# Batches 1 to 3: k is transposed inside the score passes, by a unit matrix beside the high part of q, and the channel mixer keeps two hidden buffers instead of three

## The reference

```python
def _attn_ref(q, k, v, alpha):
    for t in range(S):
        state = alpha[:, :, t, :, None] * state + np.einsum('bhd,bhe->bhde', k[:, :, t], v[:, :, t])
        y[:, :, t] = np.einsum('bhd,bhde->bhe', q[:, :, t], state)

def _moe_ref(x, w_tok1, w_tok2, w_ch1, w_ch2):      # x: (4, 768, 384)
    h = np.maximum(x.transpose(0, 2, 1) @ w_tok1, 0.0) @ w_tok2      # 768 -> 256 -> 768
    u = x + h.transpose(0, 2, 1)
    return u + np.maximum(u @ w_ch1, 0.0) @ w_ch2                    # 384 -> 1536 -> 384

def _moe2_ref(x, mu_k, mu_r, w_k, w_v, w_r):
    xk, xr = (mu * x + (1.0 - mu) * x_prev for mu in (mu_k, mu_r))
    k = np.maximum(xk @ w_k, 0.0)
    return 1.0 / (1.0 + np.exp(-(xr @ w_r))) * (k * k @ w_v)
```

## Time and profile before

| | us |
|---|---|
| median of 3 runs | 725.66 |
| lowest and highest | 725.64, 725.91 |
| the profiled execution | 725.77 |
| its span, first to last instruction | 723.8 |
| busy in the span: PE, DVE, ACT, POOL | 718.9, 474.7, 324.6, 199.8 |

### The profile page before, as it was taken

How to read it: one execution, slowest core, us unless ns; L and a number is a source line. 1 busy time by engine, 2 the same in 40 slices (tenths; PEclk the granted TensorE clock), 3 DMA queues, 4 the chain that set the end, 5 groups by cost and what they waited for, 6 DMA issues and landing times.

```text
span 723.8 us, 12708 instructions
## 1 busy us (share of the span) xinstructions
PE 718.9 (99%) x4230; PEld 676.2 (93%) x4230; DVE 474.7 (66%) x1252; ACT 324.6 (45%) x892; POOL 199.8 (28%) x351
## 2 busy tenths in 40 slices
PE   8999999999999999999999999999999999999998
PEld 7999999999999999999999999998888888888898
DVE  8988888865988875888884412348474655647361
ACT  5876554433544442544443231337353543527160
POOL 4876564333343332334432440220000000000000
PEclk9999999999999999999999999999999999999999
DMA  9975535542425544343531323012121112120201
GB/s 205 233 148 83 93 58 111 79 72 67 55 42 86 104 80 69 59 56 58 111 63 24 98 88 121 34 44 77 23 57 24 30 53 35 45 44 1 44 0 44
DMA packets 240751, 50.99 MB, mean 70 GB/s; under 512 B 221936, under 2 KB 237872, under 8 KB 240688
## 3 DMA queue, kind: packets, MB, share of 16 engines
q1 hardware_dynamic: 237408, 45.06, 33.4%
q0 software_dynamic: 1280, 4.72, 1.8%
q10 hardware_dynamic: 2000, 0.41, 0.3%
HBM read 37.17 MB, written 12.98 MB: 69 GB/s over the span
## 4 chain that ended last, share of the span: by engine, by line
PE 98%; DVE 1%; issue 0%; ACT 0%; POOL 0%; DVEq 0%; POOLq 0%
PE bank L879 21%; PE bank L895 21%; PE bank L961 14%; PE bank L983 11%; PE bank L791 5%; PE bank L970 4%; PE bank L759 4%; PE bank L867 4%; PE bank L832 3%; PE bank L1005 2%; PE bank L796 2%; PE bank L789 2%; PE bank L754 1%; PE bank L716 1%; PE bank L848 1%; PE bank L992 1%
## 5 line engine op out<-in xcount | busy, mean ns | idle before, releaser
L1108 ACT ACTIVATE hid_hi<-bank 128x384 fp32r<-128x384 f32 x96 | 47.2, 492 | 117.5 <-PE bank L879 117.4
L1391 DVE SCALAR_TENSOR_TENSOR hid_lo<-bank,hid_hi 128x384 fp32r<-128x384 f32 x96 | 53.3, 555 | 67.9 <-ACT hid_hi L1108 67.1
L879 PE MATMUL bank<-u_hi,wch_hi 128*128 128x384 f32 x288 | 72.0, 357 | 0.0
L879 PE MATMUL bank<-u_lo,wch_hi 128*128 128x384 f32 x288 | 65.9, 336 | 0.0
L895 PE MATMUL bank<-hid_lo,wch_hi 128*128 128x384 f32 x288 | 65.6, 335 | 0.0
L879 PE MATMUL bank<-u_hi,wch_lo 128*128 128x384 f32 x288 | 65.6, 335 | 0.0
L895 PE MATMUL bank<-hid_hi,wch_hi 128*128 128x384 f32 x288 | 65.4, 334 | 0.0
L895 PE MATMUL bank<-hid_hi,wch_lo 128*128 128x384 f32 x288 | 65.4, 334 | 0.0
L625 POOL TENSOR_SCALAR_AFFINE_SELECT relu_k<-relu_k 128x256 f32<-128x256 f32 x72 | 29.5, 409 | 111.2 <-ACT relu_k L1090 111.2
L1081 ACT ACTIVATE x_hi<-bank 128x96 fp32r<-128x96 f32 x96 | 23.6, 246 | 78.3 <-PE bank L796 65.4
L1305 DVE SCALAR_TENSOR_TENSOR qs_lo<-qkd,rhead,qs_hi 96x128 fp32r<-96x128 f32 x144 | 50.8, 392 | 10.1 <-ACT qs_hi L1102 8.7
(11 more groups left out here) (198 smaller groups left out, 1739.9 us busy)
## 6 DMA issues: line engine op xcount, KB each, us to landing
w_raw<-in_moe_w_ch SPq DMA_DIRECT2D x12, 384.0 KB, 3.7
vt<-in_v SPq DMA_DIRECT2D x48, 72.0 KB, 2.2
x_scratch<-x_sum SPq DMA_DIRECT2D x18, 192.0 KB, 2.1
x_sum<-x_scratch SPq DMA_DIRECT2D x72, 48.0 KB, 2.2
out<-x_half SPq DMA_DIRECT2D x40, 64.0 KB, 1.9
qka_words<-in_alpha SPq DMA_DIRECT2D x49, 48.0 KB, 2.3
qka_words<-in_k SPq DMA_DIRECT2D x49, 48.0 KB, 2.2
qka_words<-in_q SPq DMA_DIRECT2D x49, 48.0 KB, 2.3
```

The costliest lines, as they stand in the source:

```text
L879: mm = nc.tensor.matmul(dst, ch1_w(a, n % KC, jj), u[c][:, n % KC, half * HT:(half + 1) * HT], start=(n == 0), stop=(n == 3 * KC - 1))
L1108: nc.scalar.activation(dst, b_ring[t % 2][:, 0:HT], func).then_inc(tile_hi, 1)
L1391: ins = nc.vector.scalar_tensor_tensor(dst, src, 0.0, hi, ALU.max, ALU.subtract)
```

## The change

`turn_k` is gone. A unit matrix of 96 x 96 is written once by ACT at the start, between the two buffers of q's high part: `qs_hi_unit` holds q of even steps (256 words), the unit matrix (96), q of odd steps (256). In the two passes that have q's high part as the moving operand, the operand is now 352 words wide, q and the unit matrix together: even steps with q first, odd steps with the unit matrix first. The products of k's high and of k's low part with the unit matrix add up in bank 1 to k transposed, beside the scores (columns 0 to 255 and 256 to 351, or, for odd steps, 96 to 351 and 0 to 95). The middle pass, and all three for chunk 5, stay at 256 columns. `scores_done` comes from the last score pass in every step. The hidden buffers are two (HJ = 2); `hid_flat` is declared with 1024 words per part instead of 1152.

```diff
--- before.py
+++ after.py
@@ -42,7 +42,7 @@
     KT = TOK // P
     NJ = CH // P
     NF = FF // P
-    HJ = 3
+    HJ = 2
     TM = HT // P
     UNITS = 2 * NJ
     TILES = KT + 2 * KC + UNITS
@@ -99,7 +99,8 @@
         x = [sb(f"x_{n}", [P, NC, DM], F32R) for n in ("hi", "lo")]
         h1 = [sb(f"h1_{n}", [P, KT, DM], F32R) for n in ("hi", "lo")]
         u = [sb(f"u_{n}", [P, KC, S], F32R) for n in ("hi", "lo")]
-        hid = [sb(f"hid_{n}", [P, HJ, HT], F32R) for n in ("hi", "lo")]
+        hid_flat = [sb(f"hid_{n}", [P, (KC - 1) * UT], F32R) for n in ("hi", "lo")]
+        hid = [words[:, 0:HJ * HT].rearrange("p (j t) -> p j t", j=HJ) for words in hid_flat]
         x2_half = [sb(f"x2_half{n}", [P, KC, HT]) for n in range(2)]
 
 
@@ -113,7 +114,21 @@
         rhead = sb("rhead", [P, 4, 2])
         qkd = sb("qkd", [P, 6, P])
 
-        qs = [sb(f"qs_{n}", [P, 2, 2 * P], F32R) for n in ("hi", "lo")]
+        qs_hi_unit = sb("qs_hi_unit", [P, 2 * 2 * P + W2], F32R)
+        qs_lo = sb("qs_lo", [P, 2, 2 * P], F32R)
+        unit = qs_hi_unit[0:W2, 2 * P:2 * P + W2]
+
+        def qs_of(n, i):
+
+            if n == 1:
+                return qs_lo[0:W2, i % 2, :]
+            first = (2 * P + W2) * (i % 2)
+            return qs_hi_unit[0:W2, first:first + 2 * P]
+
+        def qs_and_unit(i):
+
+            first = 2 * P * (i % 2)
+            return qs_hi_unit[0:W2, first:first + 2 * P + W2]
         ks = [sb(f"ks_{n}", [P, 2, P], F32R) for n in ("hi", "lo")]
         relu_k = sb("relu_k", [P, 2, HT])
         am = relu_k[:, :, 0:2 * P]
@@ -141,7 +156,6 @@
         relu_ring, mixed_ring = ([words[:, :, :].rearrange("p a c -> p (a c)")[:, 0:UT] for words in pair]
                                  for pair in ((relu_k, decays), (mixed, qkd)))
         x_flat = [x[n][:, :, :].rearrange("p a c -> p (a c)") for n in range(2)]
-        hid_flat = [hid[n][:, :, :].rearrange("p a c -> p (a c)") for n in range(2)]
         mix_out = [[[x_flat[n][:, c * UT:(c + 1) * UT] for c in range(KC)] for n in range(2)],
                    [[x_flat[n][:, KC * UT:(KC + 1) * UT]] + [hid_flat[n][:, c * UT:(c + 1) * UT] for c in range(KC - 1)]
                     for n in range(2)]]
@@ -182,7 +196,9 @@
 
         def scores_kdT(r, i):
 
-            b_sc = bank[7] if is_first(r) and i % 2 else bank[1]
+            if not is_first(r) and i % 2:
+                return bank[1][:, W2:W2 + 2 * P], bank[1][:, 0:W2]
+            b_sc = bank[7] if i % 2 else bank[1]
             return b_sc[:, 0:2 * P], b_sc[:, 2 * P:2 * P + W2]
 
         def y_kv(r, i):
@@ -217,6 +233,7 @@
         split_ready = sem("split_ready")
         qkd_ready = sem("qkd_ready")
         scores_done = sem("scores_done")
+        unit_ready = sem("unit_ready")
         am_ready = sem("am_ready")
         am_copied = sem("am_copied")
         ks_lo_ready = sem("ks_lo_ready")
@@ -755,17 +772,15 @@
                 else:
                     pe.wait_ge(split_ready, 2 * (STEPS * (r - 1) + i + 1))
                     pe.wait_ge(ks_lo_ready, STEPS * (r - 1) + i + 1)
+                    if r == 1 and i == 0:
+                        pe.wait_ge(unit_ready, 1)
                     for n, (a, b) in enumerate(PASSES):
-                        mm = nc.tensor.matmul(scores, ks[a][0:W2, i % 2, :], qs[b][0:W2, i % 2, :],
-                                              start=(n == 0), stop=(n == 2))
-                if is_first(r) or c == NC - 1:
-                    mm.then_inc(scores_done, 1)
-
-            def turn_k(r, i):
-
-                if step(r, i)[0] < NC - 1:
-                    nc.tensor.transpose(scores_kdT(r, i)[1], qkd[0:W2, second_of(i), :], ident[0:W2, 0:W2])\
-                        .then_inc(scores_done, 1)
+                        if b == 0 and c < NC - 1:
+                            dst, moving = bank[1][:, 0:2 * P + W2], qs_and_unit(i)
+                        else:
+                            dst, moving = scores, qs_of(b, i)
+                        mm = nc.tensor.matmul(dst, ks[a][0:W2, i % 2, :], moving, start=(n == 0), stop=(n == 2))
+                mm.then_inc(scores_done, 1)
 
             def v_of(r, i):
 
@@ -815,8 +830,6 @@
                     attention_scores(r, sc)
                 if yo is not None:
                     attention_out(r, yo)
-                if sc is not None:
-                    turn_k(r, sc)
 
             def claim(b, t):
 
@@ -1098,7 +1111,7 @@
                     nc.scalar.activation(ks[0][0:W2, i % 2, :], qkd[0:W2, second_of(i), :], ACT.Copy)\
                         .then_inc(ks_hi_ready, 1)
                 for h in range(2):
-                    dst = qbd[:, i % 2, :] if is_first(r) else qs[0][:, i % 2, :]
+                    dst = qbd[:, i % 2, :] if is_first(r) else qs_of(0, i)
                     nc.scalar.activation(dst[0:W2, h * P:(h + 1) * P], qkd[0:W2, first_of(i), :], ACT.Copy,
                                          scale=rhead[0:W2, i % 4, h:h + 1])\
                         .then_inc(qbd_ready, 1)
@@ -1166,6 +1179,8 @@
             for head, stop, loaded in ((2, 4, second_pair_loaded), (4, H, qka_loaded[0])):
                 act.dma_start(qka3[0][1][:, head:stop, 0:D], k[0, head:stop, 0:P, :].rearrange("h p d -> p h d"))\
                    .then_inc(loaded, 16)
+            act.wait_ge(consts_g, 3)
+            nc.scalar.activation(unit, ident[0:W2, 0:W2], ACT.Copy).then_inc(unit_ready, 1)
             for s in range(SLOTS):
                 head_part(s)
                 for j in range(2 * CH1_END):
@@ -1302,8 +1317,8 @@
                 for h in range(2):
                     cols = slice(h * P, (h + 1) * P)
                     dve.wait_ge(qbd_ready, 2 * (STEPS * r + i) + h + 1)
-                    nc.vector.scalar_tensor_tensor(qs[1][0:W2, i % 2, cols], qkd[0:W2, first_of(i), :],
-                                                   rhead[0:W2, i % 4, h:h + 1], qs[0][0:W2, i % 2, cols],
+                    nc.vector.scalar_tensor_tensor(qs_of(1, i)[:, cols], qkd[0:W2, first_of(i), :],
+                                                   rhead[0:W2, i % 4, h:h + 1], qs_of(0, i)[:, cols],
                                                    ALU.mult, ALU.subtract).then_inc(split_ready, 1)
 
             def mask(r, i):
```

## The result

| us | before | changed |
|---|---|---|
| median (9 runs each, same chip) | 725.67 | 727.19 |
| lowest and highest | 725.62, 726.02 | 725.76, 729.09 |
| ratio, 95% interval | | 1.0019, 1.001 to 1.0027 |
| the profiled execution | 725.77 | 725.91 |
| its span | 723.8 | 724.0 |

The changed kernel is 1.52 us slower at the median, just over the 1.45 us (0.2%) that the prediction called no change (by the ratio, 1.0019, just under it). It is above the prediction's range (724.4 to 726.2), and on the other side of zero from its 0.74 us gain. The medians hide a second difference: nine executions of the kernel before lie within 0.40 us, nine of the changed one within 3.33 us. The highest of these, 729.09, also has the lowest granted clock, 0.997; the other eight lie within 1.92 us at 0.999 or more. A sum over PE's instructions can't give such a spread.

The account below looks back on a forecast made before the run. PE's own instructions were taken to bound the kernel. Removing transposes gives 5.66 us, added columns cost 4.92, net 0.74 less: 725.03 from the profiled 725.77, or 724.9 against the median; range 724.4 to 726.2.

Parts of the forecast that it names:

- What else moves: Side effects on waits, buffers, unit matrix and queues: no wait added inside the batches, SP, DVE and POOL queues keep order.
- Rival (D): A stall appears as the output step starts 0.08 later: at worst 4.8 us more, 730; chance 0.02.
- The net of the sum: Transposes removed less columns added in batches 1 to 3: 5.66 - 4.92 = 0.74 us less.
- 42 transposes behind the state product, 0.087 each: Removed transposes that follow L796, the state update: 42 x 0.087 = 3.65 us back.
- 9 behind the heads' output (first chunk), 0.11 each: Removed transposes following L791 in a head pair's first chunk: 0.99 us back, between bounds of 0.087 and 0.115 each.
- 9 in slots without an output step, 1.02 us: Removed transposes directly behind a score pass: 7 x 0.12 + 2 x 0.09 = 1.02 us back.
- The added columns, 0.041 each: 96 more columns on two of three score passes: 120 x 0.041 = 4.92 us more (4.8 to 5.04).
- The third step of batches 2 and 3: The wide first pass fills a 0.07 us hole before the second; some 0.04 either way, twice.
- the clock and the busy share of the batches: In batches 1 to 3 PE is busy throughout, 350 us, at a granted clock of 1.00.
- the two hidden buffers at nothing: ACT's writes to the hidden buffers: PE's order already frees each buffer in time, so two cost nothing.
- the unit matrix at nothing: One ACT copy of 96 x 96 at the start, 0.26 us, covered; 0.3 us once if not.
- the weighing of the rule on weight loads: Skill rules give 42.5 ns (2.4 us more in all) or 107 ns (1.5 less) per transpose; rows lie between.

Follow-up runs that it names:

- experiment 1: The changed kernel again without any edit, for more executions: 727.17 us (725.67 to 727.90, 11 runs), ratio 1.0018.
- experiment 2: The changed kernel with 120 idle instructions on PE (waits long satisfied) in place of the 60 removed transposes: 725.51 us, ratio 0.9997.
- experiment 5: The kernel before with 136 idle instructions on PE, so its blocks begin at the same work as in the changed kernel: 727.29 us, ratio 1.002.
- experiment 3: The kernel before with 120 idle instructions on PE, placed behind the transposes: 725.67 us, ratio 1.0.
- experiment 6: The kernel before with each of the 60 transposes replaced by two idle instructions, leaving out part of the computation: 721.42 us, ratio 0.9941.
- experiment 7: The changed kernel with the transposes kept, so only the wider passes and two hidden buffers are new against the kernel before: 729.91 us, ratio 1.0055.
- experiment 9: The changed kernel with 32 idle instructions on PE, all in batch 1: 725.59 us, ratio 0.9997.
- experiment 4: The kernel before with two hidden buffers instead of three and nothing else: 725.92 us, ratio 1.0002.

## Why the prediction was wrong

**The step that failed** is "What else moves". It went through the queues of the engines and found that SP's, DVE's and POOL's keep their order, and that no wait is added inside the batches. Both are right, but it looked for added waits nowhere else, and put them at nothing. It left out one queue: the one that brings PE's own instructions. Removing 120 of them moves every block transfer of the program, and one came to lie beside a store on whose end DVE, and behind it PE, depend. The kernel before had 0.23 us of cover there (update 16 at 411.637, DVE's tile at 411.87); the page says nothing of so small a margin, and the prediction looked for the thinnest place only inside the batches. Cost: 727.17 - 725.51 = 1.66 us by experiments 1 and 2, 727.29 - 725.67 = 1.62 by experiments 5 and 3.

**Rival (D)**, that a stall appears, got 0.02. It named the right kind of event at a place where it didn't occur: the earlier trace rows had two microseconds of cover, and no wait of PE shows there.

**The net of the sum was mis-sized too**, by less: -0.74 foretold, 4.20 - 4.29 = -0.09 by experiments 6 and 7, -0.28 and -0.16 by experiments 2 and 9, -0.18 in the stretch of the changed kernel's own trace. The first is a difference of medians of four runs each, good to a microsecond or so by their intervals; the two traces give 3.86 - 4.07 = -0.21. Without the collision the forecast would have been 0.6 us off, and 725.5 is inside the range. The terms:

*42 transposes behind the state product, 0.087 each.* By the distances between first score passes, experiment 6 against before, they are worth 60 to 120 ns, 3.30 us together, where the sum had 3.65. The slot of the earlier trace rows, experiment 6:

```profile
211.97 0.37 PE L795 MATMUL bank<-vt,relu_k 128*96 128x96 f32 x2
...
212.74 0.70 PE L879 MATMUL bank<-u_lo,wch_hi 128*128 128x384 f32 x3
213.28 0.68 PE L879 MATMUL bank<-u_hi,wch_lo 128*128 128x384 f32 x3
...
215.37 0.28 PE L759 MATMUL bank<-qs_hi,ks_hi 96*128 96x256 f32 x1
```

Near the transpose the price holds: 0.77 from 211.97 to 212.74, where it had been 0.85. But the next three passes take 0.54, not 0.52, and the slot 4.36 (4.354 by the exact starts), not 4.33. Such a small delay, 20 to 30 ns over a few of the mixer's passes behind the first, stands in some slots of every version and not in the same ones: of the six steps of a pair of heads (c = 0 to 5) it is in c = 1 and 2 before, in 3 to 5 in the changed kernel (and in experiments 2 and 9), in 1, 3 and 4 in experiment 6, in 0 and 5 in experiment 7. In experiment 6 the slots that take it on give back 60 ns, those that lose it 120, and the one that keeps it 87. What makes it and what places it stays open.

*9 behind the heads' output (first chunk), 0.11 each.* Wrong choice between the bounds. In the kernel before and in the changed one (first start of the output's four matmuls, then the mixer):

```profile
200.21 0.57 PE L791 MATMUL bank<-vt,relu_k 128*128 128x48 f32 x4
...
200.67 0.77 PE L879 MATMUL bank<-u_hi,wch_hi 128*128 128x384 f32 x3
```

```profile
200.17 0.57 PE L806 MATMUL bank<-vt,relu_k 128*128 128x48 f32 x4
200.56 0.77 PE L892 MATMUL bank<-u_hi,wch_hi 128*128 128x384 f32 x3
```

0.46 became 0.39. So 0.07 comes back here, and 53 ns over the slot in experiment 6, where the small delay takes the rest: 0.48 us instead of 0.99. The transpose's place had been priced like that of one more output matmul (L791), 0.11 from start to start; but the mixer's first matmul comes 0.05 behind the transpose in the kernel before (200.62 to 200.67) and 0.10 behind the last L806 in the changed one (200.465 to 200.563). Why it then starts later is open.

*9 in slots without an output step, 1.02 us.* The price of one was right, and yet only 0.29 us came back. The slot of the earlier trace rows, changed kernel:

```profile
177.91 0.32 PE L782 MATMUL bank<-qs_hi_unit,ks_lo 96*128 96x352 f32 x1
178.07 0.34 PE L880 MATMUL bank<-wtok_hi,h_hi 128*128 128x384 f32 x1
178.25 0.33 PE L880 MATMUL bank<-wtok_lo,h_hi 128*128 128x384 f32 x1
```

0.42 became 0.34, with a pass 0.04 wider: 0.12, as the sum said. But in slot 0 of batches 2 and 3 the token mixer behind it takes the gain back: by the code, `token_down` waits there for what ACT and DVE make of the tiles of `token_up`. The same matmuls of `token_down` in slot 0 of batch 2, in the kernel before and in experiment 6:

```profile
173.56 0.34 PE L867 MATMUL bank<-wtok_lo,h_hi 128*128 128x384 f32 x1
173.74 0.43 PE L867 MATMUL bank<-wtok_hi,h_lo 128*128 128x384 f32 x1
174.00 0.34 PE L867 MATMUL bank<-wtok_hi,h_hi 128*128 128x384 f32 x1
```

```profile
172.41 0.34 PE L867 MATMUL bank<-wtok_lo,h_hi 128*128 128x384 f32 x1
172.68 0.44 PE L867 MATMUL bank<-wtok_hi,h_lo 128*128 128x384 f32 x1
172.96 0.34 PE L867 MATMUL bank<-wtok_hi,h_hi 128*128 128x384 f32 x1
```

Such a matmul takes 0.17 to 0.18 when nothing holds it. Before, one of them took 0.26 (173.74 to 174.00); in experiment 6 two take 0.27 and 0.28. The slot as a whole came out 1 ns shorter, not some 110. In batch 3, another such slot came out 0.156 us longer in this trace, which is in the 0.29; its cause is open. These short pauses, 0.09 and 0.20 us, don't count as waits in the list of the earlier trace rows, where PE shows as busy: a matmul's modelled duration covers them. I had taken that list as proof that PE never stands.

*The added columns, 0.041 each.* In the timeline of the changed kernel the first pass takes 0.165 and the third 0.157, where both took 0.12: 0.080 for the two, 4.8 us for 60 steps, the lower end of what was foretold (4.8 to 5.04). A slot in which nothing else changed grew by less, 0.073 in experiment 7 (4.414 to 4.487 us, c = 3), which is 4.4 us for 60, and the small delay moving and the waits in the slots without output take it to the 3.86 of the trace (4.20 by the medians). The slope taken from rows on both sides of 352 columns was good to a tenth.

*The third step of batches 2 and 3* was foretold to swallow the wider pass. In the changed kernel it didn't: the distance behind the first pass was 0.19 and is 0.24. In experiment 7, with the same wide pass, it is 0.20, as foretold. In the changed kernel qs_lo is ready 0.14 us earlier than before, and the first pass starts 0.14 earlier (182.67); what holds the second pass for 0.08 more than its width there is open.

**Right** were the clock and the busy share of the batches, the two hidden buffers at nothing (experiment 4), the unit matrix at nothing (no wait of PE for it, PE's list of waits over the span is still the one entry of 1.7 us of the earlier trace rows), and the weighing of the rule on weight loads: 4.29 us over 60 are 0.072 a transpose, between the 0.0425 and the 0.107 that two sections of the Trainium skill's page "TensorE: Matmul & The Clock Gate" gave. The first of these, "Back-to-back issue gap", calls its formula that of an isolated matmul, which counts too little for narrow ones in a stream of loads and matmuls; the measured price agrees with that.

## What to carry to other kernels

An edit that changes the number of an engine's instructions moves all its later instruction blocks, so where a change should be worth nothing and costs something, or the executions of one kernel begin to scatter, compare the waits for DMAs in the two traces and look whether a block transfer has come beside one. The test is cheap: idle instructions in a number that moves the boundary away cure it, and in the number that moves it there (counted modulo 256) produce it in the old kernel. And before a gain on the bounding engine is summed, look for short pauses between its starts behind the place of the edit, since an engine that counts as busy can still be waiting for some tenths of a microsecond, and takes up there what it gained.

## What was not expected of the hardware

- A block transfer of 16384 bytes took 0.9 to 1.7 us, and beside it one of the sixteen updates of another DMA came 0.66, 1.62 and 2.11 us behind the fifteenth in three executions (the changed kernel, experiments 1 and 5); in the kernel before and in experiment 2, with the block elsewhere, all sixteen came within 0.19 us.
- In two of these three, one share of the store stopped while the block was moved and went on within 0.02 us of its end, with nothing else in flight.
- The delay varies between these three: wait of DVE 1.0, 2.0 and 2.5 us, time 725.91, 726.83 and 728.08. That this is the whole of the spread is not shown; the slowest executions of the changed kernel have no trace.
- 120 idle semaphore instructions on an engine that is busy 99% of the time cost nothing measurable (experiment 3: ratio 1.0, 0.9991 to 1.0008).
- Of two passes of the same 352 columns, the first takes 0.165 and the third 0.157, and three passes of the mixer right behind the plain float32 matmuls take 0.61 us before (213.75 to 214.36) and 0.62 in the changed kernel (213.55 to 214.17), the next three 0.52 to 0.54, with a transpose ahead of them or without.
